# Two rounds of look-ahead, all keys scaled by GpSimd, and attention's small matmuls threaded through the weight products

## The reference

```
# 1: attention with a decaying state, per head
for t in range(S):
    cur = einsum('bhd,bhe->bhde', u * k_t, v_t)
    y[t] = einsum('bhd,bhde->bhe', r_t, state + cur)
    state = w_t[..., None] * state + einsum('bhd,bhe->bhde', k_t, v_t)
# 2: x = y as (2, 768, 384)
h = gelu(x @ w_in); u, v = halves of h (512 each)
v_s = w_sg @ (layernorm(v) * g_ln) + b_sg
x = x + (u * v_s) @ w_out
# 3
h = relu(x.T @ w_tok1) @ w_tok2; u = x + h.T
out = u + relu(u @ w_ch1) @ w_ch2
```

## Time and profile before

| | |
|---|---|
| median of 3 runs | 398.46 us (398.12 to 400.21) |
| profiled execution | 400.32 us |
| its span, first to last instruction | 398.7 us |
| PE busy | 374.7 us, 94% |
| PEld busy | 332.1 us |
| DVE busy | 182.3 us |
| ACT busy | 106.2 us |
| POOL busy | 170.9 us |
| mean granted clock of TensorE | 0.974 |

### The profile page before, as it was taken

The page is one execution under the profiler, slowest core; times in us unless marked ns, Lnnn a source line. Parts: engine busy times, 40 slices in busy tenths (PEclk is TensorE's granted clock), DMA queues, the critical chain, the costliest instruction groups (busy, mean ns, idle before and its releaser), DMA issues.

```text
span 398.7 us, 7096 instructions
## 1 busy us (share of the span) xinstructions
PE 374.7 (94%) x2874; PEld 332.1 (83%) x2874; DVE 182.3 (46%) x295; ACT 106.2 (27%) x197; POOL 170.9 (43%) x175
## 2 busy tenths in 40 slices
PE   7887897985889999999999999999999999999996
PEld 7776785874679998999999999888888888888885
DVE  7865779999645430504442385632013311133110
ACT  5355552463302202733000033421003310022100
POOL 5754886866452798871799980000000000000000
PEclk9996997999889999999999999999999999999999
DMA  8998067636110202001112510000000000100001
GB/s 232 312 317 234 23 182 186 181 93 196 39 41 2 73 8 81 0 27 56 39 42 79 158 44 1 0 2 0 26 28 26 0 2 26 52 2 0 2 26 53
DMA packets 13953, 28.80 MB, mean 72 GB/s; under 512 B 1888, under 2 KB 6496, under 8 KB 13920
## 3 DMA queue, kind: packets, MB, share of 16 engines
q1 hardware_dynamic: 13920, 28.34, 23.9%
HBM read 25.98 MB, written 2.36 MB: 71 GB/s over the span
## 4 chain that ended last, share of the span: by engine, by line
PE 87%; DVE 6%; issue 3%; DMA 2%; SPq 1%; DVEq 0%
PE bank L1126 25%; PE bank L1127 24%; PE bank L1128 24%; DVE kp L928 5%; PE bank L1209 4%; PE bank L1145 3%; PE bank L1223 2%; DMA vn<-in_v_both 2%; PE bank L1154 1%; PE bank L1173 1%; PE bank L1254 1%; PE bank L1312 1%; PE bank L1160 0%; DVE suf L909 0%; SPq L374 0%
## 5 line engine op out<-in xcount | busy, mean ns | idle before, releaser
L790 ACT ACTIVATE ha_hi<-bank 128x512 fp32r<-128x512 f32 x36 | 21.5, 598 | 100.5 <-PE bank L1128 100.5
L1044 DVE SCALAR_TENSOR_TENSOR ha_lo<-bank,ha_hi 128x512 fp32r<-128x512 f32 x36 | 24.9, 692 | 49.7 <-ACT ha_hi L790 49.7
L1128 PE MATMUL bank<-u2T_hi,c_hi 128*128 128x512 f32 x108 | 42.1, 389 | 0.0
L1127 PE MATMUL bank<-u2T_lo,c_hi 128*128 128x512 f32 x108 | 42.0, 389 | 0.0
L1126 PE MATMUL bank<-ha_hi,c_lo 128*128 128x512 f32 x108 | 42.0, 389 | 0.0
L1127 PE MATMUL bank<-ha_lo,c_hi 128*128 128x512 f32 x108 | 42.0, 389 | 0.0
L1128 PE MATMUL bank<-ha_hi,c_hi 128*128 128x512 f32 x108 | 42.0, 389 | 0.0
L1126 PE MATMUL bank<-u2T_hi,c_lo 128*128 128x512 f32 x108 | 42.0, 389 | 0.0
L1126 PE MATMUL bank<-sg_hi,z_lo 128*128 128x384 f32 x96 | 33.3, 347 | 3.4 <-issue 3.4
L1128 PE MATMUL bank<-sg_hi,z_hi 128*128 128x384 f32 x96 | 32.8, 341 | 0.0
L1127 PE MATMUL bank<-sg_lo,z_hi 128*128 128x384 f32 x96 | 32.7, 340 | 0.0
(11 more groups left out here) (139 smaller groups left out, 862.1 us busy)
## 6 DMA issues: line engine op xcount, KB each, us to landing
krT<-in_kr_turned SPq DMA_DIRECT2D x12, 448.0 KB, 7.3
vn<-in_v_both SPq DMA_DIRECT2D x12, 416.0 KB, 7.9
raw<-in_moe_w_ch SPq DMA_DIRECT2D x12, 384.0 KB, 3.1
raw<-in_moe_w_sg SPq DMA_DIRECT2D x6, 384.0 KB, 4.9
out<-xr SPq DMA_DIRECT2D x8, 256.0 KB, 2.0
raw<-in_moe_w_in SPq DMA_DIRECT2D x4, 384.0 KB, 12.2
raw<-in_moe_w_tok SPq DMA_DIRECT2D x4, 384.0 KB, 3.0
wz<-in_w_turned SPq DMA_DIRECT2D x6, 225.8 KB, 7.1
```

The source lines that it names most:

```text
L790: sc.activation(ha[0][:, i, :], bank[:, :], ACT.Relu).then_inc(act_out, 1)
L1044: ve.scalar_tensor_tensor(ha[1][:, i, :], bank[:, :], 0.0, ha[0][:, i, :].bitcast(F32), ALU.max, ALU.subtract).then_inc(dve_out, 1)
L1127: te.matmul(dst, left[0], right[1], start=False, stop=False)
L1128: return te.matmul(dst, left[0], right[0], start=False, stop=last)
```

## The change

- `backward` and `forward` of round n + 2 are run in round n (they were spread: `forward(n + 1)` and `backward(n + 2)`); a ring of three (RR) holds rp in place of two.
- `scale_k` is GpSimd's in every round, as `scale(n + 2)`, which scales k and r together; DVE's version is gone.
- In rounds 0 to 4 `diagonal` writes bank 7 in place of bank 2, stands ahead of the state, and `keep_busy` between the blocks is gone.
- From round 5 on PE runs `diagonal` inside the last product but one of the round, two small matmuls behind each of its big ones once three big ones are through; and `outputs` and `state_products` inside the last product of the round, four small ones behind each big one.
- SLOT holds 15 products ahead of TAIL, not 18: `sg` 1 to 3 come first in TAIL.
- ACT's order in a round is: copy kn, split a weight piece, read out all products, copy the state, and `normal` for the v products of the round before.

The diff, cut to its core:

```
+RR = 3
-    (7, 0): [("v", 0, 3)], (7, 1): [("v", 0, 4)], (7, 2): [("u", 0, 4)],
-    (10, 0): [("sg", 0, 0)], (10, 1): [("sg", 0, 1)],
+    5: [("u", 0, 0), ("u", 0, 2), ("v", 0, 0)],
+    6: [("v", 0, 1), ("v", 0, 2)],
+    7: [("v", 0, 3), ("v", 0, 4)],
+    8: [("v", 0, 5), ("u", 0, 4)],
+    9: [("u", 0, 6), ("u", 0, 1)],
+    10: [("u", 0, 3), ("u", 0, 5)],
+    11: [("u", 0, 7), ("sg", 0, 0)],
...
+        def dg_bank(n):
+            return ps[7] if n < YR else b2
...
         @block.gpsimd
+            def scale(n):
+                if n < NCH:
+                    scale_k(n)
+                    scale_r(n)
             def chunk(n):
                 for b, i in v_jobs(n - 1):
                     rstd_tile(b, i)
                 if n + 1 < NCH:
                     rk_products(n + 1)
+                if n == YR:
+                    xt_low(PRE)
                 if n - 1 < NC:
                     xt_low(n - 1)
                 for piece in low.get(n, []):
                     split_low(*piece)
+                scale(n + 2)
                 for b, i in v_jobs(n - 1):
                     z_low(b, i)
...
         @block.scalar
             for n in range(YR, NCH):
                 if n % NC < NC - 1:
                     take_k(n)
...
+                for piece in high.get(n, ()):
+                    split_high(*piece)
+                for job in round_jobs(n):
+                    if "A" in OUT_BY[job[0]]:
+                        take_job(*job)
+                if n > YR and n % NC < NC - 1:
+                    take_state(n)
                 for b, i in v_jobs(n - 1):
                     normal(b, i)
...
         @block.vector
             for n in range(YR):
                 mask(n, 0)
                 mask(n, 1)
-                forward(n + 1)
-                diagonal(n)
+                backward(n + 2)
+                forward(n + 2)
                 if n:
                     y_tile(n - 1)
+                diagonal(n)
                 if n == YR - 1:
                     count_range()
-                backward(n + 2)
                 state(n)
...
-                if n + 1 < NCH:
-                    forward(n + 1)
-                    scale_k(n + 1)
-                take_slot(n, 0)
+                if n + 2 < NCH:
+                    backward(n + 2)
+                    forward(n + 2)
+                for b, i in v_jobs(n - 1):
+                    stats(b, i)
                 diagonal(n)
                 y_tile(n)
                 x_tile(n)
...
         @block.tensor
+            def three(dst, left, right, first, last, side=(), pace=0):
+                for l, r in ((1, 0), (0, 1), (0, 0)):
+                    ins = te.matmul(dst, left[l], right[r], start=first and l == 1, stop=last and (l, r) == (0, 0))
+                    for _ in range(pace):
+                        next(side, None)
+                return ins
...
+            for n in range(YR):
+                scores(n)
+                turn_kp(n)
+                rest_of(diagonal(n))
+                if n:
+                    carry_state(n)
+                rest_of(state_products(n))
+                if n == YR - 1:
+                    sum_range()
+                rest_of(outputs(n))
+            for n in range(YR, NCH):
+                scores(n)
+                if n % NC < NC - 1:
+                    turn_kp(n)
+                *before, last = round_jobs(n)
+                side = itertools.chain(itertools.repeat(None, 6), diagonal(n))
+                for t, job in enumerate(before):
+                    product(*job, side, 2 if t == len(before) - 1 else 0)
+                rest_of(side)
+                side = itertools.chain(outputs(n), state_products(n)) if n % NC < NC - 1 else outputs(n)
+                product(*last, side, 4)
+                rest_of(side)
```

More of the change, by code:

```diff
@@ L82 @@
         + [("ch1", 2, i) for i in range(NCF)] + [("ch2", 2, i) for i in range(KC)])
-ORDER = [j for n in range(NCH) for s in range(3) for j in SLOT.get((n, s), [])] + TAIL
+ORDER = [j for n in range(NCH) for j in SLOT.get(n, [])] + TAIL
 EARLY = len(ORDER) - len(TAIL)
@@ L188, in build @@
     st = put("st", [PART, NP, D])
[L189 removed]
+    t1 = put("t1", [PART, C])
     ucol = put("ucol", [PART, NP])
@@ L355, in bank_of, with round_jobs @@
             return ps[JOB[job][3]]
-        def slot_jobs(n, s):
-            return SLOT.get((n, s), [])
+        def round_jobs(n):
+            return SLOT.get(n, [])
         def v_jobs(n):
-            return [(b, i) for s in range(SLOTS) for kind, b, i in slot_jobs(n, s) if kind == "v"]
+            return [(b, i) for kind, b, i in round_jobs(n) if kind == "v"]
         def vf_tile(b, tc):
@@ L636, in split_gated @@
                                  ).then_inc(g_split, 1)
-            low = {6: [("w_in", 1), ("w_sg", 0)], 7: [("w_sg", 1)], 8: [("w_sg", 2), ("w_sg", 3)],
-                   9: [("w_sg", 4)]}
-            first = {10: [("w_sg", 5)]}
+            low = {6: [("w_in", 1)], 7: [("w_sg", 0), ("w_sg", 1)], 8: [("w_sg", 2)], 9: [("w_sg", 3)],
+                   10: [("w_sg", 4)], 11: [("w_sg", 5)]}
+            def scale(n):
+                if n < NCH:
+                    scale_k(n)
+                    scale_r(n)
             def chunk(n):
-                for piece in first.get(n, []):
-                    split_low(*piece)
                 for b, i in v_jobs(n - 1):
@@ L1122, in _ @@
             te = nc.tensor
-            def three(dst, left, right, first, last):
-                te.matmul(dst, left[1], right[0], start=first, stop=False)
-                te.matmul(dst, left[0], right[1], start=False, stop=False)
-                return te.matmul(dst, left[0], right[0], start=False, stop=last)
+            def three(dst, left, right, first, last, side=(), pace=0):
[4 more added lines that the diff above has]
+                return ins
             def cut(t, *index):
@@ L1245, in free_bank, with product @@
                     pe.wait_ge(kn_copied, states(NCH - 1))
-            def product(kind, b, i):
+            def product(kind, b, i, side=(), pace=0):
                 free_bank((kind, b, i))
@@ L1314, in _, with rest_of @@
             pe.wait_ge(ident_made, 1)
+            def rest_of(side):
+                for _ in side:
+                    pass
             keep_busy(9)
             keep_busy(4, ps[6])
-            for n in range(NCH):
+            for n in range(YR):
+                scores(n)
+                turn_kp(n)
+                rest_of(diagonal(n))
+                if n:
+                    carry_state(n)
[3 more added lines that the diff above has]
+                rest_of(outputs(n))
+            for n in range(YR, NCH):
                 scores(n)
@@ L1320, in _ @@
                     turn_kp(n)
-                if 0 < n < YR:
-                    carry_state(n)
-                if n < YR:
-                    keep_busy(2 if n else 3, ps[6] if n == 0 else ps[7])
-                for job in slot_jobs(n, 0):
-                    product(*job)
-                if n < YR:
-                    state_products(n)
-                diagonal(n)
-                if n == YR - 1:
-                    sum_range()
-                outputs(n)
-                for job in slot_jobs(n, 1):
-                    product(*job)
-                if n >= YR and n % NC < NC - 1:
-                    state_products(n)
-                for job in slot_jobs(n, 2):
-                    product(*job)
+                *before, last = round_jobs(n)
[6 more added lines that the diff above has]
+                rest_of(side)
             for job in TAIL:
```

146 lines of the change are left out of this document (60 added, 86 removed), and 5 rows, old and new, of the table SLOT.

## The result

The changed kernel takes 435.3 us (median of 4 runs, 434.1 to 441.6); the kernel before, measured beside it, 398.4 us (398.1 to 400.2). The ratio is 1.091, with a 95% interval from 1.086 to 1.095; the slow run of 441.6 us is not in it. The direction was forecast, the size was not: 408 us, and a range to 417.

A forecast was written before the change was run, and what follows sets the result against it. PE's idle time and lost clock in rounds 5 to 11 were taken as recoverable, PE then bounding them. The terms -19.1 - 1.3 + 22.5 + 6.4 + 1.5 gave +10.0 us, so 408 us, range 388 to 417.

The forecast's parts named there:

- waits and slow stretches given back: Rounds 5 to 11: PE's 13.1 us idle and 6.0 us lost to the low clock all return, -19.1 us.
- `keep_busy`, rounds 0 to 4: Removing the `keep_busy` matmuls between blocks, 2.2 us in all, gives back 1.3 us, between 0 and 3.
- threading: 98 groups of small matmuls between big ones, 0.21 us of switching each, replace 12 blocks: +22.5 us of PE work.
- late kn: Rounds 7 to 10: PE waits for ACT's kn copy behind one or two `normal` calls, +6.4 us.
- slow clock: One stretch of PE at 1.2 GHz behind a wait for kn, +1.5 us, 0 to 3.
- Rival 3: Switching between big and small matmuls on PE costs 0.31 us a group: 417 us; chance 0.15 for over 414.
- 1 (switching hidden, 388): Switching costs nothing when big and small groups alternate on PE: -10.3 us, 388 us; chance 0.25.
- Rival 2: ACT reaches its kn copy by 2.6 us after the scores start, so no wait: +2.1 us, 400.5 us; chance 0.15.

The follow-up runs named there:

- with one wait: Against the threaded kernel with kn copied early: two `normal` calls put ahead of round 8's kn alone; 433.0 us.
- with waits and blocks: Against the changed kernel: `diagonal`, `outputs` and `state_products` as blocks in place of threads, kn still copied late; 388.5 us.

## Why the prediction was wrong

Step by step, against the span's 33.9 us:

| term | predicted | found | from |
|---|---|---|---|
| waits and slow stretches given back | -19.1 | about -19 | taken over: in rounds 5 to 11 PE waits for kn alone |
| `keep_busy`, rounds 0 to 4 | -1.3 | -1.5 | scores of round 5 at 42.06, before 43.59 |
| threading | +22.5 | +32 | 0.54 us a group, 98 groups, less 21.1 |
| late kn | +6.4 | +4.5 | three waits, rounds 7 to 9 |
| slow clock | +1.5 | +17.5 | rounds 8 to 10 against 13.3, 13.0, 13.0 |
| sum | +10.0 | +33.5 | span: +33.9 |

The first row isn't measured by itself. The kernel in blocks with early kn bears it out: from the scores of round 5 to the end it needs 384.1 - 43.12 = 341.0 us against 398.7 - 43.59 = 355.1, so 14.1 less, and some 20 less without its own 3.0 us of waits and 2.7 of slow clock. The second row is no more than one execution: in the experiments, whose rounds 0 to 4 are the same, the scores of round 5 began at 42.6 to 44.8.

**The step that failed is "I add 1.5 us for one such stretch, 0 to 3."** That a wait can put PE on 1.2 GHz was seen: it happened behind the one of 2.65 us. It doesn't happen behind each wait of such a length, as the prediction had read it; in the kernel before one of 2.43 us was followed by scores at full clock, and what tells the two apart stays open:

```profile
92.67 1.16 PE L1145 MATMUL bank<-rp,kp 48*128 48x128 f32 x16 [2.43 <-DVE kp L928]
```

The length of the slow stretch was taken from the kernel before, where blocks of plain big matmuls bring the clock back; the change takes just those blocks away. The runs show both halves of it: with one wait and threads 20.1 us, with waits and blocks a clock of 0.91 in one window of 20 us, that is 1.8 us at most. The bound "0 to 3" came from the nearest row, but that row stood in the order that was being removed. This step alone carries 16 of the 24 us.

**The threading was mis-sized,** 0.55 us a group for 0.43 to 0.48. The block's own rows held part of the answer. From 47.82 to 50.36 are 2.54 us for 80 records; at the pace of `diagonal`, 24 in 0.68 us, they take 2.27. The other 0.27 us are the switch there and back, where I had taken 0.21 from the two edges, and in the threaded order it is 0.33. Why it is dearer there than at a block isn't shown. Rival 3, at 0.31 us a switch, was nearer: its threading term comes to 31.1. As a whole it still gave 417, since it too had the clock at 1.5.

**The new wait was right in kind,** with its engine, lines, rounds 8 and 9, and the two `normal` calls. It was too long: round 10 had none and round 9 only 0.97 us, because at 1.2 GHz PE comes to `diagonal` later (4.3 us behind the start of scores in round 9, 2.6 in round 8). The slow clock hid part of the wait that had caused it.

**What was given back was right** as far as the kernels with kn early bear it out (no DVE kp, GpSimd's twelve at 1.18 us each, PE busy for 279.5 of the 282 us from 150 us on). The run with kp alone moved took 10.3 us less than the median of the kernel before, and nothing less than that kernel's fastest runs; how the 19.1 us divide among the edits is thus not settled. In blocks not all of it is had, for new waits stand in rounds 9 and 10.

Of the rivals, 1 (switching hidden, 388) is out: the cost shows in every group. Rival 2 (kn in time, 400.5) can be held against the kernel with early kn: its span is 12.7 us over that of the kernel before, where the rival had +2.1. Of the 10.6 us between, 9.5 are the threading by the table.

## What to carry to other kernels

- A stall's price is the stall and the slow stretch that can follow it, and how long that stretch was depended here on what ran next. Before costing a reordering of PE's work, ask whether the new order has a run of plain big matmuls behind each place where PE can wait.
- The cost of going between the whole array and column groups is counted by the number of changes. Take it from the whole of an existing block (start of the last big one to start of the next, less the known parts), leave no remainder, and treat it as a lower bound: it gave 0.27 us here, the threads 0.33.
- A change with several parts can hide a good one: here the look-ahead and the scaling on GpSimd, with blocks and early kn, take 384.8 us, and the whole change took 435.3. Test parts alone, and when the difference of two totals gives a price, look whether the longer kernel has also lost a wait.

## What was not expected of the hardware

- The threaded order holds 2.4 GHz through the 90 us of rounds 5 to 11 when nothing interrupts it, and, after one wait of 2.65 us, runs at 1.2 GHz for 44 us with PE busy by the record. Two levels of speed for one instruction stream, chosen by one event.
- In blocks the clock came back 5.4 us after round 9's scores began, and 5.3 us into a run of big matmuls in the kernel before with kp on GpSimd (below: 3.4 us of wait, then 0.52 us each, and 0.34 from 105.25 on).

```profile
99.74 0.66 PE L1127 MATMUL bank<-sg_hi,z_lo 128*128 128x384 f32 x1 [3.41 <-issue]
100.20 0.52 PE L1128 MATMUL bank<-sg_lo,z_hi 128*128 128x384 f32 x1
...
105.00 0.41 PE L1128 MATMUL bank<-sg_lo,z_hi 128*128 128x384 f32 x1
105.25 0.34 PE L1129 MATMUL bank<-sg_hi,z_hi 128*128 128x384 f32 x1
```

- In the threaded order it did come back in the end, in round 10, in the changed kernel and in that with one wait alike: behind scores, transposes and four big matmuls, with groups already begun. Round 9 begins with the same rows and did not bring it back. Why the one and not the other stays open.
- The kernel before has two kinds of run: 387.2 to 389.0 us in three of the 29 on record, 396.2 to 401.6 in the others, and its profile is of the second kind. The one with kp on GpSimd lay within 2.3 us, at the first. Whether the varying is that of DVE's kp, let through or not, wasn't settled.
